# Re-timing the recurrence's pieces inside the first expert layer of an mLSTM and two feed-forward layers

## The chip, the cores and the metric

One core of one Trainium2 chip runs the whole program. The metric is device microseconds of one execution. The kernel before takes 455.93 us, the median of three runs (455.91 to 456.17). The profiled execution took 456.17 us; its span, from the first to the last recorded instruction, is 454.4 us.

## The reference

```python
def _attn_ref(q, k, v, i_gate, f_gate, o_gate):     # B, H, S, D = 2, 8, 768, 40
    for t in range(S):
        m_new = np.maximum(f_gate[:, :, t] + m, i_gate[:, :, t])
        f_stab, i_stab = np.exp(f_gate[:, :, t] + m - m_new), np.exp(i_gate[:, :, t] - m_new)
        C = f_stab * C + i_stab * outer(v_t, k_t)
        n = f_stab * n + i_stab * k_t
        y[:, :, t] = sigmoid(o_gate_t) * (C @ q_t) / np.maximum(np.abs(n @ q_t), 1.0)
...
x = y as [1536 tokens, 320]
x = (sigmoid(x @ w_gate) * (x @ w_val)) @ w_out               # d_ff 1536
xn = x / sqrt(mean(x * x) + 1e-6) * rms_g
g = xn @ w_gate2
out = (g * sigmoid(g) * (xn @ w_val2)) @ w_out2
```

## The kernel before, in words

The recurrence over 768 positions is cut into six chunks of 128 positions for each of the two batch rows, so there are twelve steps n = 0 to 11 (batch row n % 2, chunk n // 2). A step is a list of pieces, each of which names work on several engines:

- D: the decay weights. TensorE makes their logarithms in two banks, ScalarE takes the exponential, GpSimd scales the values (`vk`).
- S: TensorE multiplies keys by queries (32 small matmuls) into the same two banks, VectorE weighs them by the decays (`weigh`), ScalarE takes the sigmoid of the output gate.
- I: TensorE applies the carried state to the queries. K: TensorE makes the new state's increment, VectorE copies it out (`update`), GpSimd adds it. N: TensorE multiplies the weights by the values, VectorE adds the carried part (`combine`).
- Y: VectorE divides and gates (`divide`) and so makes `y_tok`.
- T: TensorE transposes the result, ScalarE rounds it into `x_hi`, VectorE makes the rest `x_lo`. These are the inputs of the first feed-forward layer. O is the same for the second layer's inputs.
- A, F, R: rows of running gate sums for a group of chunks (`PARTS`): A is VectorE's part in five bits, F a pair of transfers that lays the sums flat for D, R the column form of the sums, which TensorE transposes into bank 7 and ScalarE exponentiates into `ecol` and `gcol`. R3 serves chunks 4 and 5, that is steps 8 to 11.

The two feed-forward layers keep each fp32 operand as a rounded high part and a low part, and multiply three combinations. The first layer works on two steps' tokens at a time (a block, k = 0 to 3). A block has 16 slots: twelve `hidden` slots of 16 matmuls (gate and value for 128 hidden units), then four half projections (`project`). After the slot's own work every engine carries out the pieces that `WEAVE[k][slot]` names, in the order of the list. WEAVE is written out by hand; nothing computes it. Each engine walks the same table in its own program: TensorE in L1143 to L1151, ScalarE in L634 to L646, VectorE in L871 to L880, GpSimd in L504 to L512. In a slot ScalarE first takes the sigmoid of that slot's gate (L619) and rounds the slot before (`h_high`, L625); VectorE forms the product (`gate`, L855) and the low part of the slot before (`h_low`, L859); then both do the pieces. In block 0 ScalarE and GpSimd also split the first layer's weights into high and low parts (`high`, `split`, L533, L435, L440, L449), at the slots of `SPLIT_AT`.

Ahead of the blocks TensorE runs a start-up program by itself (L1121 to L1142): matmuls on zeros (`idle`, 128x512, bf16) between the first pieces. The engines' own start-up programs hold the same pieces: on ScalarE D0, D1, S0, S1, F1, the last third of `d_lhs` (L607, which gives the third `fill_done`), T0, T1, D2, R1.

What each piece waits for on TensorE: D of a later step waits for three `fill_done`, for `lhs_done`, for its flat rows (`flat_in`) and for the `weigh` of the step before (L925 to L929). I waits, among others, for `x_done` of the step before (L977). T waits for `y_done` (L1012). I, R and O share bank 7, and `seven` (L904 to L913) makes each of them wait for what read the one before it in the table's order (`IN_SEVEN`): after an R it is `r_exp`, the end of ScalarE's exponential of that R; after an O it is `x2_done`. The sigmoid and the exponential need different activation tables; the copy and the square do not ask for another one than is loaded.

After block 3 the second layer follows in three blocks with 512 tokens each (`hidden_pair`, `project`), with no pieces but O.

Of the kernel before, what the change touches and what calls it, by code (L numbers as in the profile page):

```python
# [10 lines left out]
B, H, S, D = 2, 8, 768, 40  # L11
# [5 lines left out]
R = B * H  # L17
# [33 lines left out]


WEAVE = [
# [19 lines left out]
def mlstm_moe_kernel(nc, gates, qk_t, vok, w_gv, w_o, rms_g, out):  # L73
# [5 lines left out]
    with ctx:  # L79
# [107 lines left out]
        bank = [ctx.enter_context(nc.psum_tensor(f"bank{i}", [P, 512], F32)) for i in range(8)]  # L187
# [710 lines left out]
        def _(pe):  # L898
# [225 lines left out]
            def idle(ps, count):  # L1124
                for _ in range(count):
                    pe.matmul(ps[:, :], zeros[:, 0:P], zeros, start=True, stop=True)

            idle(bank[6], 20)
            idle(bank[3], 1)
            for kind in "DS":  # L1130
                for n in range(B):
# [4 lines left out]
                piece(("K", n))  # L1136
            idle(bank[7], 4)
            piece(("T", 0))
            idle(bank[7], 3)
            piece(("T", 1))  # L1140
            piece(("D", 2))
            piece(("R", 1))  # L1142
            for k in range(NB0):  # L1143
                for slot in range(NF + 4):
# [73 lines left out]
```

## Time and profile before

| what | value |
|---|---|
| median of three runs | 455.93 us |
| profiled execution | 456.17 us |
| its span | 454.4 us |
| TensorE busy | 446.2 us, 98% |
| VectorE busy | 222.6 us, 49% |
| ScalarE busy | 189.7 us, 42% |
| GpSimd busy | 101.4 us, 22% |
| mean granted TensorE clock | 0.999 |

Times in the rows count from the span's start. In a timeline each row is a start, a length, an engine, a line of the kernel, an operation, what it writes and reads, the shapes and the number of instructions merged; the bracket at the end is the idle time of that engine before it and what ended it. TensorE's matmuls are pipelined: a 128x256 matmul is listed with 0.28 us, but the next one starts 0.12 us later.

### The profile page before, as it was taken

The numbers are of one execution on the slowest core, as the hardware profiler recorded it, in microseconds if no ns is written. First come the engines' busy times: TensorE is split into PE (matmuls) and PEld (weight loads), VectorE is DVE, ScalarE is ACT, GpSimd is POOL, SyncE is SP. The second block draws the span as 40 slices with busy tenths as digits, with TensorE's granted clock in tenths as the row PEclk, the third lists the DMA queues.
The fourth block names the chain that finished last, engine by engine and source line by source line (L and its number), as shares of the span: only waits on it lengthen the run. The fifth ranks groups of instructions, "written<-read, shape, count | busy, mean of one in ns | idle before, by whom it ended". The sixth has DMA issues, their size and how long they took to land.

```text
span 454.4 us, 10559 instructions
## 1 busy us (share of the span) xinstructions
PE 446.2 (98%) x4487; PEld 404.6 (89%) x4489; DVE 222.6 (49%) x465; ACT 189.7 (42%) x357; POOL 101.4 (22%) x141
## 2 busy tenths in 40 slices
PE   8898999999999999999999999999999999999997
PEld 3698999999999999998889988889988899888897
DVE  8758866772666256512543217652036640146520
ACT  8896537574456454214545134331022320123310
POOL 2989810111011010011758263000000000000000
PEclk9999999999999999999999999999999999999999
DMA  7574510121211020300334110000000001000000
GB/s 257 192 261 134 170 47 1 32 75 45 76 51 57 29 61 20 139 1 2 106 104 140 44 45 1 1 0 30 30 2 0 1 5 40 16 2 1 0 30 29
DMA packets 10127, 25.91 MB, mean 57 GB/s; under 512 B 1376, under 2 KB 4480, under 8 KB 10080
## 3 DMA queue, kind: packets, MB, share of 16 engines
q1 hardware_dynamic: 9760, 25.15, 17.2%
q8 instruction: 35, 0.57, 0.5%
q10 hardware_dynamic: 320, 0.08, 0.1%
q14 instruction: 12, 0.10, 0.1%
HBM read 23.18 MB, written 1.97 MB: 55 GB/s over the span
## 4 chain that ended last, share of the span: by engine, by line
PE 91%; DVE 6%; ACT 1%; issue 1%; DMA 0%; SPq 0%; DVEq 0%; ACTq 0%
PE bank L1098 36%; PE bank L1114 10%; PE bank L1116 9%; PE bank L1115 9%; PE bank L1047 7%; PE bank L1048 7%; PE bank L1050 4%; PE bank L965 2%; PE bank L996 2%; PE bank L901 2%; PE bank L984 1%; DVE h_lo L859 1%; PE bank L941 1%; DVE step L777 1%; PE bank L1008 1%
## 5 line engine op out<-in xcount | busy, mean ns | idle before, releaser
L619 ACT ACTIVATE sg<-bank 128x256 f32<-128x256 f32 (+1 forms) x96 | 46.9, 489 | 144.2 <-PE bank L1098 98.9
L1098 PE MATMUL bank<-x_hi,wgv_hi 64*128 64x512 f32 x576 | 105.8, 388 | 0.0
L1098 PE MATMUL bank<-x_lo,wgv_hi 64*128 64x512 f32 x480 | 93.8, 386 | 0.0
L855 DVE TENSOR_TENSOR hf<-sg,bank 128x256 f32<-128x256 f32 (+1 forms) x96 | 53.1, 553 | 60.5 <-ACT sg L619 57.6
L1047 PE MATMUL bank<-x_hi,wgv_hi 128*128 128x256 f32 x288 | 80.3, 290 | 0.3 <-DVE x_lo L814 0.3
L1048 PE MATMUL bank<-x_lo,wgv_hi 128*128 128x256 f32 x288 | 78.3, 282 | 0.0
L1114 PE MATMUL bank<-wo_hi,h_hi 128*128 128x320 f32 x240 | 75.4, 314 | 0.0
L1098 PE MATMUL bank<-x_hi,wgv_lo 64*128 64x512 f32 x384 | 75.1, 386 | 0.0
L1116 PE MATMUL bank<-wo_hi,h_lo 128*128 128x320 f32 x240 | 74.2, 309 | 0.0
L1115 PE MATMUL bank<-wo_lo,h_hi 128*128 128x320 f32 x240 | 74.1, 309 | 0.0
L853 DVE TENSOR_TENSOR sg<-sg,bank 128x512 f32<-128x512 f32 x36 | 24.8, 688 | 85.8 <-ACT sg L619 83.7
L1098 PEld LDWEIGHTS bank<-x_hi,wgv_hi 64*128 64x128 f32 x576 | 54.4, 184 | 11.5 <-issue 0.7
L1047 PEld LDWEIGHTS bank<-x_hi,wgv_hi 128*128 128x128 f32 x288 | 55.0, 191 | 1.4 <-issue 0.5
L1048 PEld LDWEIGHTS bank<-x_lo,wgv_hi 128*128 128x128 f32 x288 | 55.1, 191 | 0.0
L1050 PE MATMUL bank<-x_hi,wgv_lo 128*128 128x256 f32 x192 | 54.3, 283 | 0.0
L1098 PEld LDWEIGHTS bank<-x_lo,wgv_hi 64*128 64x128 f32 x480 | 45.4, 184 | 8.9
L859 DVE TENSOR_TENSOR h_lo<-hf,h_hi 128x256 fp32r<-128x256 f32 (+1 forms) x84 | 51.7, 615 | 0.2
L1114 PEld LDWEIGHTS bank<-wo_hi,h_hi 128*128 128x128 f32 x240 | 45.1, 188 | 1.5 <-issue 1.1
L625 ACT ACTIVATE h_hi<-hf 128x256 fp32r<-128x256 f32 (+1 forms) x84 | 42.3, 504 | 9.5 <-DVE hf L855 9.3
L1115 PEld LDWEIGHTS bank<-wo_lo,h_hi 128*128 128x128 f32 x240 | 45.1, 188 | 0.0
L1116 PEld LDWEIGHTS bank<-wo_hi,h_lo 128*128 128x128 f32 x240 | 45.1, 188 | 0.0
L1098 PEld LDWEIGHTS bank<-x_hi,wgv_lo 64*128 64x128 f32 x384 | 36.3, 184 | 7.3
(129 smaller groups left out, 560.9 us busy)
## 6 DMA issues: line engine op xcount, KB each, us to landing
step<-in_vok SPq DMA_DIRECT2D x12, 324.0 KB, 3.0
step<-in_qk_t SPq DMA_DIRECT2D x24, 160.0 KB
step<-in_w_gv SPq DMA_DIRECT2D x6, 576.0 KB, 3.8
raw_p<-in_w_gv SPq DMA_DIRECT2D x5, 576.0 KB, 3.7
raw_x<-in_w_gv SPq DMA_DIRECT2D x5, 576.0 KB, 5.0
step<-in_vok SPq DMA_DIRECT2D x10, 160.0 KB, 4.2
raw_x<-in_w_o SPq DMA_DIRECT2D x3, 480.0 KB, 3.5
raw_p<-in_w_o SPq DMA_DIRECT2D x3, 480.0 KB, 3.3
```

The lines of the kernel that those rows point to most:

```text
L619: act.activation(sg_view(n), g_view(n), ACT.Sigmoid).then_inc(sg_done, 1)
L625: act.activation(h_view(n, 0), hf_view(n), ACT.Copy).then_inc(hhi_done, 1)
L853: dve.tensor_tensor(sg_view(n), sg_view(n), g_view(n), ALU.mult).then_inc(silu_done, 1)
L855: dve.tensor_tensor(hf_view(n), sg_view(n), v_view(n), ALU.mult).then_inc(hf_done, 1)
L859: dve.tensor_tensor(h_view(n, 1), hf_view(n), h_view(n, 0).bitcast(F32), ALU.subtract).then_inc(h_done, 1)
L1047: pe.matmul(ps, wgv_hi[:, wc, s, cs], x_hi[:, xs, s, :], start=(s == 0), stop=False)
L1048: mm = pe.matmul(ps, wgv_hi[:, wc, s, cs], x_lo[:, xs, s, :], start=False, stop=(s == 2))
L1050: pe.matmul(ps, wgv_lo[:, wc, s, cs], x_hi[:, xs, s, :], start=False, stop=False)
L1098: mm = pe.matmul(ps(n), w, x, start=own and (s, p) == (0, 0), stop=last and not own)
L1114: pe.matmul(ps, h_view(n0 + f, 0)[:, ts], wo_hi[:, f, :], start=(f == 0), stop=False)
L1115: pe.matmul(ps, h_view(n0 + f, 0)[:, ts], wo_lo[:, f, :], start=False, stop=False)
L1116: mm = pe.matmul(ps, h_view(n0 + f, 1)[:, ts], wo_hi[:, f, :], start=False, stop=(f == NF - 1))
```

## The change

Three edits to the order of the work; no operation of the computation is added, removed or resized. The first edits block 0 of WEAVE: I2, K2 and N2 go from slot 3 to slot 5 and stand behind S3, which comes there from slot 6; Y2 goes from slot 4 to 6, T2 from 7 to 8, I3, K3 and N3 from 9 to 10, Y3 from 10 to 11. The second moves R3 from block 1, slot 13, to block 2, slot 4. The third edits TensorE's start-up: 23 idle matmuls in the first group in place of 20, and D2 stands between T0 and T1, with two idle matmuls behind it, in place of three idle matmuls there and D2 behind T1. ScalarE's and VectorE's start-up programs are as before. `IN_SEVEN` is built from WEAVE, so R3 now stands between O2 and I7 in it.

```diff
--- before.py
+++ after.py
@@ -51,13 +51,13 @@
 
 
 WEAVE = [
-    [[], [("S", 2)], [], [("D", 3), ("I", 2), ("K", 2), ("N", 2)], [("Y", 2)], [], [("S", 3)], [("T", 2)], [],
-     [("I", 3), ("K", 3), ("N", 3)], [("Y", 3)], [], [("A", 2, 0), ("A", 2, 1)],
+    [[], [("S", 2)], [], [("D", 3)], [], [("S", 3), ("I", 2), ("K", 2), ("N", 2)], [("Y", 2)], [], [("T", 2)], [],
+     [("I", 3), ("K", 3), ("N", 3)], [("Y", 3)], [("A", 2, 0), ("A", 2, 1)],
      [("A", 2, 2), ("T", 3), ("A", 2, 3), ("A", 2, 4)], [("F", 2)], [("R", 2)]],
     [[("D", 4)], [("O", 0), ("A", 3, 0)], [("S", 4)], [("O", 1), ("A", 3, 1)], [("D", 5)], [("F", 3)],
      [("S", 5), ("I", 4), ("K", 4), ("N", 4)], [("Y", 4)], [("A", 3, 2)], [("T", 4), ("D", 6), ("A", 3, 3), ("A", 3, 4)],
-     [], [("S", 6), ("I", 5), ("K", 5), ("N", 5)], [("Y", 5)], [("R", 3)], [("T", 5), ("D", 7)], [("F", 4)]],
-    [[("S", 7), ("I", 6), ("K", 6), ("N", 6)], [("Y", 6)], [("O", 2)], [("T", 6), ("D", 8)], [],
+     [], [("S", 6), ("I", 5), ("K", 5), ("N", 5)], [("Y", 5)], [], [("T", 5), ("D", 7)], [("F", 4)]],
+    [[("S", 7), ("I", 6), ("K", 6), ("N", 6)], [("Y", 6)], [("O", 2)], [("T", 6), ("D", 8)], [("R", 3)],
      [("S", 8), ("I", 7), ("K", 7), ("N", 7)], [("Y", 7)], [], [("T", 7), ("D", 9), ("O", 3)], [("F", 5)],
      [("S", 9), ("I", 8), ("K", 8), ("N", 8)], [("Y", 8)], [], [("T", 8), ("D", 10)], [],
      [("S", 10), ("I", 9), ("K", 9), ("N", 9)]],
@@ -1125,7 +1125,7 @@
                 for _ in range(count):
                     pe.matmul(ps[:, :], zeros[:, 0:P], zeros, start=True, stop=True)
 
-            idle(bank[6], 20)
+            idle(bank[6], 23)
             idle(bank[3], 1)
             for kind in "DS":
                 for n in range(B):
@@ -1136,9 +1136,9 @@
                 piece(("K", n))
             idle(bank[7], 4)
             piece(("T", 0))
-            idle(bank[7], 3)
+            piece(("D", 2))
+            idle(bank[7], 2)
             piece(("T", 1))
-            piece(("D", 2))
             piece(("R", 1))
             for k in range(NB0):
                 for slot in range(NF + 4):
```

## Rows read from the trace of the kernel before

**Rows 1.** The page, part 4: the chain that ended last, by engine.

```profile
PE 91%; DVE 6%; ACT 1%; issue 1%; DMA 0%; SPq 0%; DVEq 0%; ACTq 0%
```

**Rows 2.** Waits of TensorE, whole span: total us, times, longest us.

```profile
PE bank L901 <- DVE y_tok L785: 2.2, 2, 1.7
```

**Rows 3.** Timeline of TensorE, 0 to 22 us: start, length, instruction, count, idle before.

```profile
1.26 7.24 PE L1126 MATMUL bank<-inter 128*128 128x512 bf16 x21 [1.26 <-DVE inter L821]
...
8.34 0.38 PE L934 MATMUL bank<-causal,ident_b 128*128 128x512 bf16 x1
...
13.44 1.13 PE L996 MATMUL bank<-step,tail 128*64 128x41 f32 x32
...
17.77 0.81 PE L1126 MATMUL bank<-inter 128*128 128x512 bf16 x3
...
19.13 0.55 PE L901 MATMUL bank<-ident,y_tok 128*128 128x128 f32 x3 [0.54 <-DVE y_tok L785]
...
19.43 0.71 PE L941 MATMUL bank<-d_rhs,d_lhs 128*128 128x256 f32 x4
...
20.85 0.39 PE L1047 MATMUL bank<-x_hi,wgv_hi 128*128 128x256 f32 x1 [0.33 <-DVE x_lo L814]
```

**Rows 4.** Timeline of ScalarE, same stretch.

```profile
8.98 1.09 ACT L548 ACTIVATE tail<-bank 128x512 f32<-128x512 f32 x2 [0.61 <-PE bank L936]
...
16.87 1.27 ACT L607 ACTIVATE d_lhs<-num 64x1280 fp32r<-64x1280 f32 x1
```

**Rows 5.** Timeline of VectorE, same stretch.

```profile
12.28 2.47 DVE L750 TENSOR_TENSOR tail<-bank,tail 128x512 f32<-128x512 f32 x4
...
14.67 0.14 DVE L769 TENSOR_SCALAR den<-bank 128x8 f32<-128x8 f32 x1
```

**Rows 6.** Timeline of TensorE, 36 to 51 us, around the first block's stalls.

```profile
43.22 0.55 PE L901 MATMUL bank<-ident,y_tok 128*128 128x128 f32 x3 [1.69 <-DVE y_tok L785]
...
48.38 0.68 PE L984 MATMUL bank<-cst,step 40*64 40x41 f32 x32 [0.79 <-DVE x_lo L814]
```

**Rows 7.** Timeline of VectorE, 36 to 46 us, ahead of the first stall.

```profile
36.28 0.42 DVE L855 TENSOR_TENSOR hf<-sg,bank 128x256 f32<-128x256 f32 x1 [1.63 <-ACT sg L619]
...
36.62 2.09 DVE L859 TENSOR_TENSOR h_lo<-hf,h_hi 128x256 fp32r<-128x256 f32 x1
...
38.63 0.96 DVE L775 SCALAR_TENSOR_TENSOR den<-num,den 128x8 f32<-128x8 f32 x1
```

**Rows 8.** Timeline of GpSimd, 36 to 47 us.

```profile
36.42 2.00 POOL L435 TENSOR_TENSOR wgv_lo<-raw_p,wgv_hi 128x384 fp32r<-128x384 f32 x2
...
43.09 2.93 POOL L449 TENSOR_TENSOR wo_lo<-raw_x,wo_hi 128x320 fp32r<-128x320 f32 x3
```

**Rows 9.** Timeline of VectorE, 49 to 52 us: update and combine of step 3.

```profile
49.82 0.32 DVE L798 COPY cnew<-bank 104x164 f32<-104x164 f32 x1
...
51.60 0.17 DVE L769 TENSOR_SCALAR den<-num 128x8 f32<-128x8 f32 x1
```

**Rows 10.** Timeline of VectorE at 102 us, GpSimd quiet.

```profile
101.95 0.49 DVE L777 TENSOR_TENSOR step<-step,rden 128x320 f32<-128x320 f32 x1
```

**Rows 11.** Timeline of TensorE, 66 to 69 us: D of step 4.

```profile
67.60 0.28 PE L1048 MATMUL bank<-x_lo,wgv_hi 128*128 128x256 f32 x1
...
67.97 0.71 PE L941 MATMUL bank<-d_rhs,d_lhs 128*128 128x256 f32 x4
```

**Rows 12.** Timeline of TensorE at 104 us: second half of piece R3.

```profile
104.43 0.29 PE L952 MATMUL bank<-l_end,ones 16*64 16x16 f32 x4
```

**Rows 13.** Timeline of ScalarE, 60 to 72 us: piece R2's exponential.

```profile
65.24 1.28 ACT L569 ACT_TABLE_LOAD   x1 [4.25 <-issue]
...
66.54 0.20 ACT L569 ACTIVATE ecol<-bank 128x32 f32<-128x32 f32 x1
```

**Rows 14.** Timeline of ScalarE, 120 to 130 us: third block.

```profile
127.15 0.38 ACT L619 ACTIVATE sg<-bank 128x256 f32<-128x256 f32 x1
```

**Rows 15.** Timeline of TensorE, 126 to 130 us: I of step 7.

```profile
127.52 0.62 PE L984 MATMUL bank<-cst,step 40*64 40x41 f32 x32
```

## The prediction

> **What bounds the kernel now.** First the page's chain that ended last: TensorE holds 91% of it [rows 1], so a change of order is worth only what it does to TensorE's gaps, to what TensorE executes, or to the moment at which its gapless part begins. Next TensorE's waits over the span: 2.2 us in two waits for `y_tok`, the longest 1.7 [rows 2]. The timelines place them and one more: the 1.69 us stand before T2 at 43.22 and 0.79 us for `x_lo` before I3 at 48.38 [rows 6]; the rest is the start-up, before the first hidden matmul at 20.85 [rows 3]. Nothing behind 70 us waits. So there are about 2.5 us to win in block 0, and every new wait costs its full length, since nothing later could absorb it. Of the three engines that serve the pieces I read the timelines at the places that the diff touches, to see who would be late there.
>
> **Edit 3, the start-up.** The 21 idle matmuls run from 1.26 to 8.50 and D0's first matmul starts at 8.34, in their tail, not at a wait [rows 3]. Idle matmuls follow each other every 0.215 us at the higher clock level, 2.4 GHz ((0.81 - 0.38) / 2, [rows 3]), and the end of the first group already runs at it. Three more: D0 0.65 us later. Who passes that on? ScalarE waits for D0 (0.61 us idle, 8.98, [rows 4]) and then works without a gap to the end of L607 at 18.14; with 0.65 that is 18.8. On VectorE the four weighings from 12.28 (0.62 each, [rows 5]) have just enough cover: the third, S1's, starts at 13.5, and S1, which ends at 13.44 less four idles = 12.6, moves to 13.2. But TensorE's own order is S1, four idles, N0, and N0 ends at 13.44 + 1.13 = 14.57 [rows 3] while VectorE reads it at 14.67 [rows 5]: no slack, so both divisions and T1 (19.13) move by 0.65. D2, now ahead of T1, needs the third `fill_done`, which is L607's end: 18.8 + 0.65 us (19.43 to R1 at 20.08, the row's length without its pipelined tail, [rows 3]) + two idles 0.43 = 19.9 to 20.0. T1 is then held by that order rather than by `y_tok` (19.8). Behind T1 nothing is won by D2's absence: the first hidden matmul waits 1.72 us behind T1 (19.13 to 20.85) for ScalarE's and VectorE's parts, an interval that D2 and R1 sat in for nothing. Cost: 0.8 us, bounds 0 (should D0's delay be hidden somewhere) and 1.0. I take 0.8.
>
> **Edit 1, block 0.** What follows is in the old times, without the 0.8 us, which all engines share here. The pieces stay the same, so only waits count. T2 stands one hidden slot later. A slot is 2.0 us: from T2 at 43.22 to I3's arrival at 48.38 - 0.79 = 47.59 there are T2 itself and two slots [rows 6]. TensorE would reach T2 at 43.22 - 1.69 + 2.0 = 43.5. When is `y_tok` there? VectorE is idle until 36.28, where gate 4 waits for ScalarE (1.63 us, [rows 7]); ScalarE is late for the tables and exponential of D3, which stays in slot 3, so this start stays. Before, Y2 came right behind: gate 4, h_low 3, Y2 (38.63 to 43.16). Now seven things stand between h_low 3 and Y2: gate 5, h_low 4, weigh 3, update 2, combine 2, gate 6, h_low 5. The idle time that K2, I2 and N2 leave in slots 3 and 4 lies before 36.28 and is lost.
>
> Their prices: a gate 0.35 us (36.28 to 36.62). A weighing of one step 1.2 (half of 2.47, [rows 5]). Update and combine 1.6 (49.82 to 51.77 less 0.33 of waiting, [rows 9]). An instruction with both inputs in SBUF is a lottery here: h_low 3 took 2.09 us and L775 0.96, each until GpSimd's running instruction ended [rows 7, 8], while L777 took 0.49 with GpSimd quiet [rows 10]. So: h_low 3 until 37.8 (one GpSimd instruction, not two); gate 5 and h_low 4 until 38.9; weigh 1.2, update and combine 1.6, gate 6 0.4: 42.2; h_low 5 0.4; Y2 against the end of GpSimd's weight splitting, which goes on in pieces of 1 us as at 43.09 [rows 8], 3.7 us rather than the 4.5 of before: `y_tok` at 46.3. T2 then waits 46.4 - 43.5 = 2.9 us instead of 1.7. Bounds of Y2's end: 43.7 with every instruction at its quiet length (Y2 1.7 us), 47.5 with each of them a GpSimd instruction late. The wait before T2 is thus 0.2 to 4.1 us.
>
> I3 comes two slots behind T2 as before, 4.4 us; behind Y2 VectorE now has two gates, two h_lows and x_lo, 2.2 to 3.2 us, instead of these and one more pair and a weighing. The 0.8 us wait before I3 goes. Block 0's stalls: 2.9 against 2.5, +0.4 (bounds -2.3 and +1.6).
>
> Y3, in slot 11, now stands ahead of h_low 11, which the last part of the first projection needs; by the same count it is there 0.5 us ahead. VectorE's gate sums (A2) start at about the old time, while TensorE comes 0.4 later. That frees 0.25 us before D4: at 67.97 TensorE had waited for the flat rows, for without a wait D4 follows the slot's last matmul after 0.12 us, at 67.72 [rows 11]. -0.25 (bounds -0.25 and +0.5, should A2 be late).
>
> **Edit 2, R3.** On TensorE it costs 0.44 us wherever it stands (104.21 to 104.65, [rows 12]). Before, ScalarE's exponential had half a block until the next user of bank 7. Now I7 in slot 5 is the next user and `seven` makes it wait for `r_exp`. Count both. TensorE reaches I7 at 127.52 [rows 15], unchanged, for R3's 0.44 us left block 1 and came back in block 2. ScalarE's sigmoid of slot 4 starts at 127.15 [rows 14], and now 0.44 earlier, 126.71; with it and h_high 3 ScalarE is at 127.4. The sigmoid's table is loaded, so R3 needs the other: 1.28 us (as at 65.24, [rows 13]) and 0.3 for `ecol` and `gcol`: `r_exp` at 129.0. I7 waits 129.0 - 127.5 = 1.5 us. Queued behind I7 are K7, N7 and the whole hidden chain. ScalarE then loads the sigmoid's table again (1.28) ahead of slot 5's sigmoid, and VectorE's gate 5, weigh 8 and combine 7 are late, but Y7 ends some 0.5 us before the likewise delayed T7. +1.5 (bounds 0 and 2.0).
>
> The profile has ScalarE begin the exponential 0.02 us after the table load ends (65.24 + 1.28, next at 66.54, [rows 13]). The Trainium skill ("ScalarE: Activation LUTs", What ACT_TABLE_LOAD costs) speaks against this edit more strongly: 1283 ns for the load and about 1380 ns more of drain at every switch. By it I7 would wait 2.9 us, an estimate; the trace shows the load and not the drain, and I keep the trace.
>
> **Sum.** 0.8 + 0.4 - 0.25 + 1.5 = +2.45 us. The profiled execution took 456.17 us, 1.8 us more than its span, and lies 0.24 above the median; added to the median 455.93 this gives 458.4.
>
> **Rivals.**
> 1. VectorE is ahead of T2. Place: Y2's end. If its two-input instructions run at their quiet lengths, `y_tok` is there at 43.7, and the wait before T2 is 0.2 us. The total is 0.8 - 2.3 - 0.25 + 1.5 = -0.25: 455.7, not slower. It decides from Y2's end at about 44.0. For it: GpSimd leaves short gaps between its instructions. Against: its stretches of 2.0 and 2.9 us [rows 8] leave little room, and h_low 3 and L775 both ran into them [rows 7]. 10%.
> 2. R3's wait is not there, because ScalarE gets to it early: +0.95, 456.9. For it only that ScalarE is busy 42% of the span; against, the sigmoid of slot 4 is bound by the table loads of D8. 10%.
> 3. The start-up delay is absorbed: +1.65, 457.6. For it: VectorE's weighing is not delayed. Against: the 0.1 us between N0's end and its reader. 12%.
> 4. A table switch that also drains, in R3's place: 1.4 us more, 459.8. 8%.
> 5. As forecast: 50%. The rest are mixtures, rivals 1 and 2 together (454.2) among them.
>
> **How the numbers follow.** The terms' bounds add to far more than they will do together; the range reaches down to rival 2 and up to rival 4: 456.8 to 459.9, which leaves about 18% out. A measurement here tells 0.2%, 0.9 us. Slower by more: the forecast, 3, 4, about half of rival 2 and most mixtures, 0.85. Within: rival 1 and what is left of 2, 0.09. Faster: 0.06.
>
> **What would show it.** D0's first matmul at 9.0 and the first hidden one near 21.7. One wait of TensorE for `y_tok` before T2 of 2 to 4 us, none for `x_lo`. No gap before D4. In block 2 a table load right behind the sigmoid of slot 4, and TensorE idle for 1.5 us before I7 with L569's `ecol` or ScalarE as the releaser. I am wrong if T2 comes without a wait, or if I7 follows S8 at once.

## The result and the profile after

The changed kernel takes **462.74 us** (median; 462.11 to 463.72), the kernel before, timed beside it, 456.05 (455.91 to 456.48). The ratio is 1.0147, 95% interval 1.0128 to 1.0167: 6.7 us slower. The forecast was 458.4, range 456.8 to 459.9. The direction was right and the size was not: more than half of the loss, by the medians, is something that the forecast's sum did not contain.

The profiled execution took 461.69 us, with a span of 459.9 against 454.4. First the page: the row of TensorE's granted clock and the chain that ended last, which is TensorE's as in [rows 1].

```profile
PEclk9999899999989999999999999999999999999999
...
PE 92%; ACT 5%; DVE 2%; issue 1%; ACTq 0%
```

Two slices read 8: the fifth, at 46 to 57.5 us, and the twelfth, at 126 to 138. Now the waits of TensorE over the whole span (total us, times, longest us), to be held against [rows 2]:

```profile
PE bank L901 <- DVE y_tok L785: 3.9, 1, 3.9
PE bank L984 <- ACT gcol L570: 1.4, 1, 1.4
...
PE bank L1047 <- DVE x_lo L814: 0.8, 1, 0.8
PE bank L941 <- ACT d_lhs L607: 0.8, 1, 0.8
```

The two waits in front of T2 and I7 lie where the forecast had them. The timeline of TensorE in the start-up (start, length, instruction, count, idle before), which answers to [rows 3]:

```profile
1.26 7.66 PE L1126 MATMUL bank<-inter 128*128 128x512 bf16 x24 [1.26 <-DVE inter L821]
8.76 0.38 PE L934 MATMUL bank<-causal,ident_b 128*128 128x512 bf16 x1
...
18.61 0.74 PE L941 MATMUL bank<-d_rhs,d_lhs 128*128 128x256 f32 x4 [0.76 <-ACT d_lhs L607]
...
19.64 0.49 PE L901 MATMUL bank<-ident,y_tok 128*128 128x128 f32 x3
...
21.30 0.39 PE L1047 MATMUL bank<-x_hi,wgv_hi 128*128 128x256 f32 x1 [0.80 <-DVE x_lo L814]
```

The 24 idle matmuls end only 0.42 us later than the 21 did, and the hidden work starts 0.45 us later (20.85 to 21.30), not 0.8. The timeline of TensorE around the two new waits, which answers to [rows 6] and [rows 15]:

```profile
47.51 0.90 PE L901 MATMUL bank<-ident,y_tok 128*128 128x128 f32 x3 [3.95 <-DVE y_tok L785]
...
49.91 0.41 PE L1047 MATMUL bank<-x_hi,wgv_hi 128*128 128x256 f32 x1
50.13 0.38 PE L1048 MATMUL bank<-x_lo,wgv_hi 128*128 128x256 f32 x1
...
50.46 0.28 PE L1047 MATMUL bank<-x_hi,wgv_hi 128*128 128x256 f32 x1
...
53.06 0.68 PE L984 MATMUL bank<-cst,step 40*64 40x41 f32 x32
...
129.04 1.10 PE L965 MATMUL bank<-step 40*64 40x128 f32 x32
131.50 0.68 PE L984 MATMUL bank<-cst,step 40*64 40x41 f32 x32 [1.35 <-ACT gcol L570]
```

T2 waits 3.95 us, and I3 no longer waits. But behind T2 the hidden matmuls follow each other every 0.21 us until 50.3, and only then every 0.12 as everywhere else. The busy time by stretch of the changed kernel, with the granted clock in the column PEclk (0.50 is 1.2 GHz, 1.00 is 2.4 GHz):

```profile
43.50:46.90 3.40, 0.06 (x1) 0.00 (x0) 3.30 (x5) 0.85 (x2) 3.24 (x4) 1.00 0.33 128
46.90:50.30 3.40, 2.79 (x13) 2.80 (x14) 2.97 (x6) 1.80 (x3) 2.59 (x4) 0.50 0.70 182
50.30:53.70 3.40, 3.40 (x58) 3.22 (x56) 1.41 (x3) 2.12 (x5) 3.02 (x4) 0.99 0.82 244
128.90:132.30 3.40, 2.05 (x74) 1.66 (x75) 0.76 (x2) 3.34 (x7) 0.00 (x0) 0.99 0.00 0
132.30:135.70 3.40, 3.40 (x54) 3.32 (x49) 2.69 (x8) 1.29 (x4) 0.85 (x2) 0.50 0.15 17
```

The first number behind the length is TensorE's busy time. In the stretch that holds the wait before T2, TensorE was busy for 0.06 of 3.4 us; in the next one its clock was 1.2 GHz. In the stretch with the wait before I7 it was busy for 2.05 us, and again the next ran at 1.2 GHz. The same five stretches of the kernel before all have a granted clock of 1.00; here is its last:

```profile
132.30:135.70 3.40, 3.40 (x31) 3.40 (x30) 2.65 (x9) 0.94 (x4) 0.00 (x0) 1.00 0.12 18
```

The same pieces stand in both timelines, so the growth of 5.5 us can be followed from piece to piece. Each start is from the two timelines of TensorE:

| piece | before | after | later by | what changed since the row above |
|---|---|---|---|---|
| first hidden matmul | 20.85 | 21.30 | 0.45 | start-up |
| T3 | 59.56 | 62.33 | 2.77 | +2.32: waits 3.95 less 1.69 and 0.79 is +1.47; +1.18 from the clock; -0.33 is left |
| D4 | 67.97 | 70.49 | 2.52 | -0.25: the gap before D4 is gone |
| T5 | 107.39 | 109.21 | 1.82 | -0.70, nearly all of it R3's own time |
| S8 | 126.60 | 129.04 | 2.44 | +0.62: R3 is back |
| I7 | 127.52 | 131.50 | 3.98 | +1.54: I7 waits for R3's exponential |
| T7 | 135.29 | 140.81 | 5.52 | +1.54: the clock |

Behind T7 nothing more is added. The clock's 1.18 us is T2 to I3, 5.55 us against the 4.37 that the same order takes without a wait (48.38 - 0.79 - 43.22, [rows 6]). The -0.33 has a place: S3 and I2, K2, N2 now stand side by side, and TensorE changes less often between hidden and small matmuls; it came to T2 at 43.56 (47.51 - 3.95), 2.03 us later than before (43.22 - 1.69), where a slot without pieces (1.92, from 39.56 to 41.48 in the changed kernel) and the start-up (0.45) make 2.37.

This one execution fell to 1.2 GHz twice, and its mean granted clock is 0.993. A fall is 3.4 us at half, so one takes 3.4 x 0.5 / 460 = 0.004 from the mean. Three of the four timed executions had 0.989, which answers to three falls, and were at 462.11 to 463.72.

### The profile page after: what moved, and what is told of

The parts are those of the page before. It is cut to its first block, busy times and chain, and to the rows that moved or that the text cites. A ratio compares the mean times of both kernels' runs of the same rounds, so it can differ in the third digit from the quotient of the medians.

```text
span 459.9 us, 10566 instructions
## 1 busy us (share of the span) xinstructions
PE 448.9 (98%) x4491; PEld 408.5 (89%) x4491; DVE 219.7 (48%) x465; ACT 192.7 (42%) x359; POOL 101.0 (22%) x141
## 4 chain that ended last, share of the span: by engine, by line
PE 92%; ACT 5%; DVE 2%; issue 1%; ACTq 0%
PE bank L1098 36%; PE bank L1114 9%; PE bank L1116 9%; PE bank L1115 9%; PE bank L1047 7%; PE bank L1048 7%; PE bank L1050 4%; PE bank L996 2%; PE bank L965 2%; PE bank L1126 2%; PE bank L901 2%; ACT wgv_hi L533 1%; PE bank L984 1%; ACT tail L548 1%; PE bank L941 1%
## 5 line engine op out<-in xcount | busy, mean ns | idle before, releaser
L855 DVE TENSOR_TENSOR hf<-sg,bank 128x256 f32<-128x256 f32 (+1 forms) x96 | 53.1, 553 | 68.9 <-ACT sg L619 66.3
L1047 PE MATMUL bank<-x_hi,wgv_hi 128*128 128x256 f32 x288 | 81.4, 293 | 0.8 <-DVE x_lo L814 0.8
L859 DVE TENSOR_TENSOR h_lo<-hf,h_hi 128x256 fp32r<-128x256 f32 (+1 forms) x84 | 50.6, 603 | 0.0
```

The source lines that it names most:

```text
L855: dve.tensor_tensor(hf_view(n), sg_view(n), v_view(n), ALU.mult).then_inc(hf_done, 1)
L859: dve.tensor_tensor(h_view(n, 1), hf_view(n), h_view(n, 0).bitcast(F32), ALU.subtract).then_inc(h_done, 1)
L1047: pe.matmul(ps, wgv_hi[:, wc, s, cs], x_hi[:, xs, s, :], start=(s == 0), stop=False)
```

## The experiments

The theory after the two traces: the waits of the forecast are there, and the rest is the clock, which falls behind a wait and costs some microseconds more. The rival: the loss is in the waits and the order alone, and the low clock in the trace is an accident of this execution. The first four kernels take the edits apart and take the clock away. Where the granted clock of single executions is given, 1.000 means no fall, 0.996 one, 0.993 two. This is worked out from the mean; where such a fall lay is known only for the profiled executions.

**One edit at a time.** e1_startup_only is the kernel before with the start-up's edit alone:

```diff
-            idle(bank[6], 20)
+            idle(bank[6], 23)
...
-            idle(bank[7], 3)
-            piece(("T", 1))
             piece(("D", 2))
+            idle(bank[7], 2)
+            piece(("T", 1))
```

> Edit 3 alone on the kernel before. Theory A (each long wait of TensorE costs its length, and the clock fall to 1.2 GHz behind it costs 1.5 to 1.7 us more; the start-up edit has neither): D0 later, first hidden matmul 0.4 to 0.8 us later, T2 and I3 waits as before (1.7 and 0.8 us), no stretch at half the clock, +0.5 us in the median (0.3 to 0.9). Rival B (the start-up edit shifts something that brings the clock falls): a stretch of 3.4 us at half the clock appears here, +2 us or more.

Measured: 456.65 us (455.97 to 457.7), ratio 1.0012 (1.0003 to 1.002). Ten of its eleven executions kept the clock; they spread from 455.97 to 457.7, where the kernel before spreads from 455.93 to 456.66. The 0.35 us over the 456.3 of the kernel before is near the 0.45 us of the trace. The profiled one, 457.28, had a fall of its own, at the start of the hidden work. Its wait of TensorE for a transfer and its stretches:

```profile
PE bank L941 <- DMA d_rhs<-l_row: 1.2, 1, 1.2
```

```profile
18.10:21.50 3.40, 1.86 (x14) 1.36 (x14) 1.68 (x5) 1.16 (x3) 3.24 (x4) 0.99 0.56 173
21.50:24.90 3.40, 3.17 (x15) 3.17 (x16) 0.64 (x3) 3.30 (x7) 1.77 (x2) 0.50 0.92 284
```

There D2 waited for the landing of its flat row, and the clock fell behind that. D2 stands ahead of T1 now, so whatever holds D2 holds all.

e2_block0_only is the kernel before with block 0's new order alone (the first change in the diff of WEAVE, two lines against two):

> Edit 1 alone on the kernel before. Theory A: T2 waits some 3.5 to 4 us for y_tok, the wait before I3 goes, the clock falls once for 3.4 us near 46 us; +0.4 to +1.2 us of waits, -0.4 us of fewer switches and the D4 gap, +1.5 of clock, together +2 to +3 us. Rival B (the fall hangs on the start-up's phase or on the sum of waits): no fall, +0.3 to +1.2 us.

Measured: 459.1 us (458.28 to 459.36), ratio 1.0058 (1.0046 to 1.007), so +2.8. Two executions at 0.996 took 458.3 and 458.4, three at 0.993 took 459.1 to 459.4. The longest wait for `y_tok` is 3.9 us, and the stretch behind it again runs at 0.50:

```profile
43.80:47.20 3.40, 0.29 (x3) 0.29 (x4) 3.33 (x6) 0.00 (x0) 3.24 (x4) 1.00 0.35 86
47.20:50.60 3.40, 3.40 (x19) 3.40 (x18) 2.08 (x4) 1.76 (x3) 2.84 (x4) 0.50 0.61 202
```

No execution was without a fall, and of the 17 executions of the kernel before that were timed beside it none had a mean clock under 0.999. That speaks against the rival, which takes the fall for chance. It also shows that a second fall needs neither the start-up's edit nor a wait before I7: this kernel has neither, and three of its five executions had two. Its profiled execution had one, so no trace shows where the second lay. Between its executions with one fall and those with two there are 0.9 us.

e3_r3_only is the kernel before with R3 moved alone:

```diff
-     [], [("S", 6), ("I", 5), ("K", 5), ("N", 5)], [("Y", 5)], [("R", 3)], [("T", 5), ("D", 7)], [("F", 4)]],
-    [[("S", 7), ("I", 6), ("K", 6), ("N", 6)], [("Y", 6)], [("O", 2)], [("T", 6), ("D", 8)], [],
+     [], [("S", 6), ("I", 5), ("K", 5), ("N", 5)], [("Y", 5)], [], [("T", 5), ("D", 7)], [("F", 4)]],
+    [[("S", 7), ("I", 6), ("K", 6), ("N", 6)], [("Y", 6)], [("O", 2)], [("T", 6), ("D", 8)], [("R", 3)],
```

> Edit 2 alone on the kernel before. Theory A in the strict form (only a wait of about 4 us brings the clock down, the second fall was an echo of the first): I7 waits 1.4 us, +1.5 us and no fall. Theory A': the 1.4 us wait among S8, I7, K7 and N7, whose matmuls are small, is enough by itself: +3.0 us with one stretch of 3.4 us at half the clock near 130 us.

Measured: 458.13 us (457.82 to 461.06), ratio 1.0055 (1.0036 to 1.0074). Four executions kept the clock and took 457.8 to 458.15, one had a mean of 0.996 and took 459.08, one 0.993 and 461.06. The wait before I7 is 1.35 us here too, in the profiled execution, which kept the clock, and the edit costs 1.8 us then. So four of six executions went by this wait without a fall; that the falls of the other two lay behind it is likely, and no trace shows it.

The three edits with the clock as it came: 0.35 + 2.8 + 1.83 = 5.0 us of 6.7. Together they cost more than singly. The mean clocks fit that: two or three falls in each execution of the changed kernel, none as a rule in e1 and e3, one or two in e2.

**The clock taken away.** e4_fillers_in_waits is the changed kernel, with matmuls that compute nothing needed in the two waits, 6 ahead of I7 and 17 ahead of T2: TensorE is kept busy while it would stand still.

```diff
+            def fill(ps, count):
+                for _ in range(count):
+                    pe.matmul(ps[:, :], ident_b[:, :], causal[:, :].unsqueeze(1).to_broadcast([P, 4, P]), start=True, stop=True)
...
+                    if n == 7:
+                        pe.wait_ge(x_done, n)
+                        fill(bank[6], 6)
...
+                    if n == 2:
+                        pe.wait_ge(p_done, 8)
+                        fill(bank[4], 17)
```

> The changed kernel with matmuls without use in the two waits: 17 of 128x512 (3.7 us) ahead of T2's wait for y_tok, 6 (1.3 us) ahead of I7's waits. Their results are overwritten. Theory A (the clock falls because TensorE's array stands idle): both falls go, no wait gets longer, the kernel is 3.0 to 3.4 us faster than the changed one, +2.2 to +3.5 us over the kernel before. Rival B (the falls do not come from these waits): both stay, the time is as the changed kernel's, +5.5 to +6.7.

Measured: 458.8 us (458.6 to 461.5), ratio 1.0055 (1.0042 to 1.0068). The pieces start when they did, VectorE and ScalarE are as late as they were, and TensorE has 23 matmuls more to do; and the kernel is 3.9 us faster than without them (462.7 to 458.8). Four executions at a clock of 1.000 took 458.6 to 458.9. The stretches that ran at 0.50 in the changed kernel, and the one behind T2's wait, which comes 2.5 us later here (T2 starts at 49.99):

```profile
46.90:50.30 3.40, 2.79 (x16) 1.24 (x14) 3.33 (x6) 0.00 (x1) 3.24 (x4) 1.00 0.45 131
49.40:52.80 3.40, 2.81 (x24) 2.82 (x25) 2.84 (x6) 2.01 (x5) 2.00 (x3) 1.00 0.84 208
...
132.30:135.70 3.40, 3.40 (x91) 2.90 (x89) 1.50 (x4) 2.50 (x6) 0.46 (x1) 1.00 0.02 5
```

The rival is out. With the clock kept the change costs 458.7 - 456.3 = 2.4 us, and the forecast's sum was 2.45. (The profiled execution, 461.5, had a fall at the start of the hidden work, behind a wait of 1.5 us for D2's flat row.) The changed kernel and e4 were timed at different times, each beside the kernel before (456.05 and 456.3); by the differences to it the fillers win 4.2 us, by the medians as they stand 3.9.

**One filler at a time.** f1_filler_t2 has the 17 matmuls before T2 only, f2_filler_i7 the 6 before I7 only; the edit is that of e4, halved.

> The changed kernel with the 17 matmuls ahead of T2's wait only; I7's wait stays bare. Theory A: the fall near 46 us goes, the one behind I7 stays or not with the run (it was absent in half the runs with edit 2 alone); 459.5 to 461 us in the median, a granted clock of 0.996 or 1.0. Rival B (the second fall is the whole loss): as the changed kernel, 462 to 463.

> The changed kernel with the 6 matmuls ahead of I7's waits only. Theory A: the fall near 46 us stays (one stretch, sometimes two, as with edit 1 alone), none behind I7: 460.5 to 461.5 us. Rival B (a fall there carries on a weakness from the one at 46 us, not I7's wait): a fall near 132 us still there.

Measured: f1 460.4 us, ratio 1.0105 (1.0089 to 1.012), three executions of 460.3 to 460.5 at 0.996 and one of 462.2 at 0.993. Its profiled execution ran throughout at a mean clock of 0.754 and took 551 us; it is left out of the median, and no row of it is read. f2 460.73 us (460.16 to 461.0), ratio 1.01 (1.0087 to 1.0114), three at 0.996 and one at 0.992. With both fillers it was 458.7 at 1.000, with one 460.2 to 461.0 at 0.996. A fall thus costs 1.5 to 2.3 us here, 1.2 and 1.5 in the profiled execution of the changed kernel, and 0.9 to 1.0 between the executions of e2 and e3. The fall that is left in f2 lies behind T2's wait, as its profiled execution shows (48.0 to 51.4 at 0.50), and behind I7 there is none (134.8 to 138.2 at 1.00), so the 6 fillers do keep the clock there. The one that is left in f1 should be that behind I7's wait, but no usable trace shows it; if it is, that wait brought a fall in every timed execution of f1 and in two of six of e3 at most.

**What makes y_tok late.** In the forecast VectorE's two-input instructions run against GpSimd's weight splitting. g_gpsimd_light is the changed kernel with less of it: of layer one, GpSimd's splits of the last two chunks of the first weight and of the whole second weight are cut to 8 columns, and their low parts are zeros, so this kernel leaves out part of the correction terms. Zeroing them delays the start: D0 waits 2.3 us for it, and the first hidden matmul starts at 24.65, 3.35 us later than in the changed kernel.

```diff
+                w = slice(0, 8) if lay == 0 and c >= 6 else slice(0, CW)
...
-                    pool.tensor_tensor(wgv_lo[:, c, s, :], r[:, s, :], wgv_hi[:, c, s, :].bitcast(F32),
+                    pool.tensor_tensor(wgv_lo[:, c, s, w], r[:, s, w], wgv_hi[:, c, s, w].bitcast(F32),
...
+                    w = slice(0, 8) if lay == 0 else slice(0, DM)
```

> The changed kernel, with GpSimd's weight splits from the seventh weight chunk of layer one on cut to 8 of 384 or 320 columns (the low parts of those weights are left out otherwise, and set to zero in the start-up), so that GpSimd is nearly idle while VectorE works towards Y2. It tells what makes T2 wait. Theory A (half the list, half GpSimd): y_tok comes at 44.5 to 45.5 instead of 47.5, T2's wait falls from 3.9 to 1.0 to 2.0 us, the fall near 46 us goes, the kernel gains 3 to 4 us. Rival B (the length of VectorE's list alone): y_tok no earlier than 46.5. Rival C (GpSimd alone): no wait at T2.

Measured: 460.16 us (458.85 to 464.36), ratio 1.0106 (1.0063 to 1.0148), with 3.35 us of late start in it. Two executions kept the clock and took 458.85 and 459.0, two had falls (0.992 and 0.985) that no trace places. Less the late start, the first two would stand at 455.6, an estimate. The timelines say more. First VectorE of the changed kernel, from gate 4 to the end of Y2:

```profile
36.68 0.42 DVE L855 TENSOR_TENSOR hf<-sg,bank 128x256 f32<-128x256 f32 x1 [4.51 <-ACT sg L619]
37.02 1.12 DVE L859 TENSOR_TENSOR h_lo<-hf,h_hi 128x256 fp32r<-128x256 f32 x1
...
43.00 1.32 DVE L775 SCALAR_TENSOR_TENSOR den<-num,den 128x8 f32<-128x8 f32 x1
...
44.59 0.99 DVE L777 TENSOR_TENSOR step<-step,rden 128x320 f32<-128x320 f32 x1
...
46.51 0.94 DVE L785 TENSOR_TENSOR y_tok<-num,step 128x128 f32<-128x128 f32 x1
```

And of g_gpsimd_light (its lines are numbered 4 higher):

```profile
40.03 0.42 DVE L859 TENSOR_TENSOR hf<-sg,bank 128x256 f32<-128x256 f32 x1 [4.51 <-ACT sg L623]
40.37 0.42 DVE L863 TENSOR_TENSOR h_lo<-hf,h_hi 128x256 fp32r<-128x256 f32 x1
...
45.77 0.16 DVE L779 SCALAR_TENSOR_TENSOR den<-num,den 128x8 f32<-128x8 f32 x1
...
46.20 0.49 DVE L781 TENSOR_TENSOR step<-step,rden 128x320 f32<-128x320 f32 x1
...
47.07 0.29 DVE L789 TENSOR_TENSOR y_tok<-num,step 128x128 f32<-128x128 f32 x1
```

From gate 4 to the end of Y2 it is 10.8 us with GpSimd at work (36.68 to 47.45) and 7.3 without (40.03 to 47.36). T2 then waits 0.5 us instead of 3.9, less than the 1.0 to 2.0 that theory A had. So with the new order and a quiet GpSimd 0.5 us of the wait is left. That does not make the order harmless: the next kernel has the old order with GpSimd at work, and there T2 in slot 8 does not wait at all. The wait needs both, and either alone takes nearly all of it away. The Trainium skill ("GPSIMD Engine Reference", Specifications) says that GpSimd shares its SBUF interfaces with VectorE, with contention for VectorE instructions that have two inputs in SBUF. The trace agrees: L777 takes 0.49 us in quiet and 0.99 here, while L855, with one input in PSUM, takes 0.42 in both.

**T2 later, without the rest.** If the wait is the price of seven instructions ahead of Y2, then T2 one slot later with Y2 left where it was should win what the changed kernel was to win. h_t2_later_only is the kernel before with block 0 so:

```diff
-    [[], [("S", 2)], [], [("D", 3), ("I", 2), ("K", 2), ("N", 2)], [("Y", 2)], [], [("S", 3)], [("T", 2)], [],
-     [("I", 3), ("K", 3), ("N", 3)], [("Y", 3)], [], [("A", 2, 0), ("A", 2, 1)],
+    [[], [("S", 2)], [], [("D", 3), ("I", 2), ("K", 2), ("N", 2)], [("Y", 2)], [], [("S", 3)], [], [("T", 2)],
+     [], [], [("I", 3), ("K", 3), ("N", 3)], [("Y", 3), ("A", 2, 0), ("A", 2, 1)],
```

> A candidate: the kernel before, with T2 one slot later (slot 8), I3, K3 and N3 in slot 11 and Y3 at the head of slot 12; S3, I2, K2, N2 and Y2 and the start-up and R3 as before. By theory A VectorE's list ahead of Y2 stays short, y_tok comes at 43.2 before TensorE reaches T2 at 43.5, x_lo at 49 before I3 at 49.8: no wait at either, nothing late behind, 453.5 to 454.2 us against 456.2 (-0.5%). Rival B (VectorE or GpSimd is merely late elsewhere): a new wait in the projection or at D4 eats at least 1 us.

Measured: 454.8 us (454.76 to 454.92), ratio 0.9973 (0.9961 to 0.9984). That is 1.2 us faster than before, and not the 2.0 and more that I had expected. TensorE's timeline has both stalls of block 0 gone and two new ones, 0.53 us before T3 and 0.65 us before D5, for a weighing of step 4:

```profile
43.18 0.51 PE L901 MATMUL bank<-ident,y_tok 128*128 128x128 f32 x3
49.41 0.68 PE L984 MATMUL bank<-cst,step 40*64 40x41 f32 x32
57.46 0.55 PE L901 MATMUL bank<-ident,y_tok 128*128 128x128 f32 x3 [0.53 <-DVE y_tok L785]
...
76.59 0.71 PE L941 MATMUL bank<-d_rhs,d_lhs 128*128 128x256 f32 x4 [0.65 <-DVE tail L750]
```

**Three more.** In i_a3_later, h with one more change, the first two parts of A3 (the gate sums of the last group of chunks), which stand ahead of that weighing on VectorE, come two slots later. In j_a2_before_y3 those of A2, the group before, come ahead of Y3 in addition, on top of i. In k_y2_in_slot5 the changed kernel's Y2 stands at the end of slot 5, ahead of gate 6, and T2 stays.

```diff
-    [[("D", 4)], [("O", 0), ("A", 3, 0)], [("S", 4)], [("O", 1), ("A", 3, 1)], [("D", 5)], [("F", 3)],
+    [[("D", 4)], [("O", 0)], [("S", 4)], [("O", 1), ("A", 3, 0)], [("D", 5)], [("F", 3), ("A", 3, 1)],
```

> The candidate h (454.8 us) with A3's first two parts one or two slots later in block 1 (slots 3 and 5 in place of 1 and 3). In h TensorE waits 0.65 us before D5 for the weighing of step 4, and those parts (1.2 us on VectorE) stand ahead of it. Theory A: the wait is mostly gone, 454.2 us. Rival B (the tables on ScalarE set the weighing, not VectorE's list): the wait stays at 0.5 us or more, 454.7.

Measured: **454.18 us** (454.12 to 454.79), ratio 0.9961 (0.9949 to 0.9972), every execution at a clock of 1.000. The wait before D5 is gone (D5 at 75.76 without one); the 0.53 us before T3 stay. This is the best version found: 2.0 us faster than the 456.2 of before, where the change as a whole is 6.7 slower. T2 and I3 come later, the gate sums give way to a weighing, and nothing more stands ahead of Y2.

```diff
-     [], [], [("I", 3), ("K", 3), ("N", 3)], [("Y", 3), ("A", 2, 0), ("A", 2, 1)],
-     [("A", 2, 2), ("T", 3), ("A", 2, 3), ("A", 2, 4)], [("F", 2)], [("R", 2)]],
+     [], [], [("I", 3), ("K", 3), ("N", 3)], [("A", 2, 0), ("A", 2, 1), ("Y", 3)],
+     [("A", 2, 2), ("A", 2, 3), ("T", 3), ("A", 2, 4)], [("F", 2)], [("R", 2)]],
```

> Kernel i with A2's parts ahead of Y3 and of T3's x_lo in block 0, so that the flat rows and R2 come earlier and ScalarE gets to D4 earlier. Theory A: another 0 to 0.4 us, 453.8 to 454.2. Rival B: Y3 is now late for T3 and TensorE waits for y_tok there, 454.5 or more.

Measured: 457.99 us (456.89 to 459.27), ratio 1.0041 (1.0029 to 1.0053), 3.8 us slower than i. The gate sums hold up Y3, T3 waits 2.81 us for `y_tok`, and the clock falls behind it. The timeline of TensorE and its stretches:

```profile
59.87 0.55 PE L901 MATMUL bank<-ident,y_tok 128*128 128x128 f32 x3 [2.81 <-DVE y_tok L785]
```

```profile
57.40:60.80 3.40, 0.93 (x7) 0.93 (x8) 3.22 (x11) 0.34 (x1) 0.00 (x0) 1.00 0.00 0
60.80:64.20 3.40, 3.40 (x15) 3.40 (x14) 2.41 (x6) 1.70 (x4) 1.01 (x2) 0.50 0.48 151
```

That is rival B. The same mistake at another place has the same result; 2.3 of the 3.8 us are the longer wait (2.81 against 0.53).

```diff
-    [[], [("S", 2)], [], [("D", 3)], [], [("S", 3), ("I", 2), ("K", 2), ("N", 2)], [("Y", 2)], [], [("T", 2)], [],
+    [[], [("S", 2)], [], [("D", 3)], [], [("S", 3), ("I", 2), ("K", 2), ("N", 2), ("Y", 2)], [], [], [("T", 2)], [],
```

> The changed kernel with Y2 at the end of slot 5 in place of slot 6, so that gate 6 and h_low 5 stand behind it on VectorE; all else as changed. Theory A (T2's wait is VectorE's list, drawn out by GpSimd): y_tok comes 0.8 to 1.3 us earlier, the wait before T2 falls from 3.9 to about 2.9 us; the fall of the clock behind it may stay. 461 to 462 us. Rival B (Y2 is held by something else, as ScalarE's sigmoid): y_tok as before, 47.5.

Measured: 459.28 us (458.4 to 460.77), ratio 1.0069 (1.0055 to 1.0082). T2's wait shrinks from 3.95 to 2.09 us with nothing but Y2's place changed, more than the 1.0 us that I had expected, and the time is 2 us below the 461 to 462 of the expectation. The fall behind the wait stays. Timeline and stretches of k_y2_in_slot5:

```profile
46.08 0.55 PE L901 MATMUL bank<-ident,y_tok 128*128 128x128 f32 x3 [2.09 <-DVE y_tok L785]
```

```profile
43.80:47.20 3.40, 1.31 (x12) 1.12 (x11) 3.31 (x4) 0.81 (x2) 2.88 (x4) 0.99 0.39 131
47.20:50.60 3.40, 3.40 (x19) 3.40 (x18) 2.74 (x7) 3.16 (x8) 2.67 (x3) 0.50 0.65 171
```

## Why the prediction was wrong, and where it was right

**The step that failed** is in its first part: "every new wait costs its full length". A new wait cost its full length and then a stretch at 1.2 GHz behind it. The profile before showed waits of 1.69 and 0.79 us in block 0 at a granted clock of 1.00 throughout, and I took this for the rule. In the changed kernel one wait is 3.95 us and one is 1.35 us among small matmuls, and both were followed by 3.4 us at half the clock. Neither the sum, nor the range, nor any of the rivals held a fall. The fillers of e4 show it: with the clock kept the change costs 2.4 us, without the fillers 6.7. That 2.4 is so near the forecast's 2.45 is in part luck: the start-up was put 0.35 us too high and block 0 some 0.7 too low.

**Start-up, forecast 0.8, measured 0.45.** D0 came 0.42 us later and not 0.65. The idle matmuls do not take a fixed time each: the first ones follow each other at about 0.43 us, twice the 0.215 of the later ones, until about 6.4 us in the trace before and about 6.0 in the one after. (This is worked out from 21 of them in 7.24 us and 24 in 7.66; PEclk reads 1.00 there all the same.) In five traces with the new count the 24 took from 6.88 us (e1) to 8.18 (f2), so three more of them move D0 by less or more than their length.

The way in which the 0.42 was passed on was the forecast's on ScalarE and not on VectorE. ScalarE's L607 ended 0.42 us later (18.14 to 18.56), D2 waited for it, and T1 waited behind D2 and its idles until 19.64. VectorE lost nearly all of the delay again: its first division began 0.38 us later (14.67 to 15.05), but L777 in it took 0.49 us instead of 0.82, and the second `y_tok` came 0.06 us later, at 19.13.

```profile
18.79 0.28 DVE L785 TENSOR_TENSOR y_tok<-bank,step 128x128 f32<-128x128 f32 x1
18.85 0.28 DVE L785 TENSOR_TENSOR y_tok<-bank,step 128x128 f32<-128x128 f32 x1
```

The first line is the kernel before, the second the changed one. So "both divisions and T1 move by 0.65" was wrong, and the cost comes from D2's place ahead of T1: with the old order T1 could have gone at about 19.2, an estimate. The kernels with the old start-up bear this out: their D0 starts anywhere from 7.97 (h) to 8.34 us (before), and their first hidden matmul at 20.75 to 20.85 all the same. In e1's and e4's profiled executions D2 waited 1.2 and 1.5 us for a DMA, which the forecast had not seen, and the new order passed that on too. Rival 3 (delay absorbed) was right about VectorE and wrong in the whole.

**Block 0, forecast +0.4, measured +1.14 without the clock** (1.47 of waits less 0.33). The mechanism was right: seven things of VectorE's list ahead of Y2, `y_tok` late, T2 waits, I3 does not. Y2 took 4.45 us (43.00 to 47.45), not 3.7: L775 took 1.32 us against 0.16 in quiet, and L777, L783 and L785 two to three times their quiet length. `y_tok` was there at 47.0 in old times instead of 46.3, and these 0.7 us are the whole miss of this term. I had taken the wait to be 2.9 us with bounds 0.2 and 4.1, and it was 3.95; the 0.33 us won by fewer changes between hidden and small matmuls was no term of mine and brings TensorE to T2 earlier, which makes the wait longer and costs nothing. Rival 1 (VectorE in time at quiet lengths) is what g_gpsimd_light shows: without GpSimd's work it is 7.3 us from gate 4 to Y2's end, where the quiet bound of the forecast had 7.4 (36.28 to 43.7), and its time less the late start, 455.6, is near the 455.7 of the rival. Its condition was not met in the changed kernel.

**The gap before D4, forecast -0.25, measured -0.25.** [rows 11] had read it rightly.

**R3 before I7, forecast 1.5, measured 1.54** (a wait of 1.35, and 0.19 of a longer change to the small matmuls), and 1.8 in e3. R3 itself costs 0.62 us wherever it stands, not 0.44, which cancels as forecast. Rival 2 (no wait) was wrong. Rival 4 (a table switch that also drains) was wrong, as the timeline of ScalarE shows:

```profile
129.68 1.28 ACT L569 ACT_TABLE_LOAD   x1
130.97 0.20 ACT L569 ACTIVATE ecol<-bank 128x32 f32<-128x32 f32 x1
131.07 0.18 ACT L570 ACTIVATE gcol<-bank 128x16 f32<-128x16 f32 x1
131.26 1.28 ACT L619 ACT_TABLE_LOAD   x1
132.56 0.38 ACT L619 ACTIVATE sg<-bank 128x256 f32<-128x256 f32 x1
```

The exponential starts 0.01 us after the load's end and the sigmoid 0.02 after the next. The drain of about 1380 ns of the Trainium skill ("ScalarE: Activation LUTs", What ACT_TABLE_LOAD costs) is in neither place, so the measurement decides against it.

**The sum.** Waits and order: 0.45 + 1.14 - 0.25 + 1.54 - 0.08 (left over between D4 and S8) = 2.8 us in the profiled execution, 2.4 by e4, against 2.45 forecast. The clock: 1.18 + 1.54 = 2.7 in the profiled execution, which had two falls, and 3.9 by medians (462.7 less 458.8). By medians it was the larger half.

**What stays open.** Three of the four timed executions of the changed kernel have a mean clock that answers to three falls, and no trace shows the third. The start-up is one possible place, since the profiled executions of e1 and e4 had one there; but e2, with the old start-up and nothing at I7, also had one fall more than its trace places in three of five executions, so a second fall behind the same wait, or elsewhere, is as possible. Why the 1.35 us before I7 brings a fall in some executions and not in others (e3) is open as well, and so is whether the small matmuls around it matter. A version with fillers in front of D2 would test the start-up, and was not run.

## What to carry to other kernels

A wait of the engine that sets the end has two prices, its length and the clock behind it; give every new wait a fall (here 0.9 to 2.3 us) as a term with a chance of its own, or fill the wait with matmuls that nobody needs. The longest wait that the profile before shows at full clock is no safe bound: 1.69 us kept it there, and 1.35 elsewhere did not. Before moving work behind others in a queue, count what now stands ahead of the thing that is waited for, at the lengths that it has against the other engines' work at that time and not at its quiet ones. Moving the consumers of block 0 alone (T2 one slot later, Y2 untouched) won 1.2 us, and 2.0 with A3 out of the way, where moving the producer with them lost 2.8 (e2, block 0's edit by itself).

## What the runs showed of the hardware

- Useless matmuls in two waits made the kernel 3.9 us faster (462.7 to 458.8); the clock stayed at 1.00 behind both.
- The fall is not tied to a full standstill: behind a wait of 3.95 us it came in the executions traced (T2), behind 2.81 and 2.09 too, but also behind 1.35 us among matmuls of 41 columns (TensorE busy 2.05 of 3.4 us in the changed kernel), and at the start of the hidden work in e1 and e4, whose D2 had waited 1.23 and 1.49 us. Waits of 1.69 and 0.79 us did not bring it in the kernel before, and the same 1.35 us did not in the traced execution of e3.
- Each fall in the traces lasts 3.4 us, as in 46.90 to 50.30, and then the clock is back at 1.00 without any change in the work.
- GpSimd's elementwise work under VectorE's instructions cost 3.4 of 10.8 us (g_gpsimd_light against the changed kernel).
- The time that the same 24 idle matmuls take at the start differs between executions: 6.88 to 8.18 us in five traces (e1, e4, changed, k, f2).
